# Attention and two mixture-of-experts layers: token rows scattered into one DRAM region per expert, the last rows of an expert in tiles of 64

## The chip, the cores and the metric

The program runs on one core of one Trainium2 chip. A core has TensorE (PE, matrix products, written to the eight banks of PSUM), VectorE (DVE), ScalarE (ACT), GpSimd (POOL) and SyncE (SP), each with its own instruction stream; they meet at semaphores only. All but PE can issue DMAs. The metric is the device time of one execution in microseconds (us), lower is better.

## The reference, cut to what matters

Attention with 4 batches, 8 heads, 768 positions and head size 64, a local window of 96 keys and 8 global keys, gives 3072 token rows of 512. Two layers of experts follow, each with 8 experts of 512 x 1024 and 1024 x 512; every token goes to one expert:

```python
def _moe_ref(x, w_gate, w_output_gate, w1, w2):
    logits = x @ w_gate
    e_idx = np.argmax(logits, axis=1)
    ...
    for e in range(E):
        mask = e_idx == e
        h = np.maximum(x[mask] @ w1[e], 0.0)
        ye = h @ w2[e]
        out[mask] = gate_w[mask, None] * eom[mask, e, None] * ye

def _moe2_ref(x, expert_emb, tau, w1, w2):
    xn = x / (np.linalg.norm(x, axis=-1, keepdims=True) + 1e-06)
    en = expert_emb / (np.linalg.norm(expert_emb, axis=-1, keepdims=True) + 1e-06)
    logits = xn @ en.T / tau
    expert_idx = np.argmax(logits, axis=1)
    ...
        out[mask] = gate_w[mask, None] * (h @ w2[e])
```

`gate_w` is the largest softmax probability of a token, `eom` a sigmoid of a second product. All is float32. With the inputs of this case the experts of the first layer get 455, 416, 361, 397, 367, 410, 395 and 271 tokens, those of the second 445, 228, 374, 430, 340, 278, 299 and 678.

## The kernel before

**Attention.** A batch is six tiles of 128 queries (`j`), a tile two steps (`u`) of four heads. In a step PE makes scores (L1166), DVE adds the bias and takes the maximum (L904), ACT takes the exponent (L709), PE turns the probabilities (L1126), ACT and DVE copy them out of PSUM (L721, L916), and PE multiplies them with the values (L1199). For that last product the two heads of a pair use weights of 64 columns each and write to partitions 0 to 63 and 64 to 127. Two steps later the rows of a tile are turned and normalised into `x_tok` (L876), their 16 gate logits are made (L1141, L883, L887), and ACT's queue writes them to `x_rows` in DRAM (L727). The streams are written out by hand; each engine does the same step `u` in the same order.

**Routing (`route`).** When all 24 tiles are done, DVE finds for all tokens at once the expert, the gate and the rank within the expert, with PE's help (L1217 to L1221), gives each expert whole tiles of 128 slots, and turns the token-to-slot table round with one product per token tile (L1016 to L1023, L1228). In the second layer this waits for all the tiles of the first.

**Experts.** Layer 0 has 29 tiles, layer 1 has 28. A tile on PE is, in this order: `first_product` (L1246, 32 products with 128 moving columns, which the trace lists as 64), `x_tr` of the next tile (L1126, four transposes), `second_product` (L1256, 8 products with 512 moving columns, listed as 16). POOL gathers the 128 rows of a tile by an indirect DMA into `x_g` (L632) as soon as the transposes of the tile before have read it. DVE copies the turned rows (`x_copy`, L1064), scales the result by the gate (`y_scale`, L1075), and in layer 0 makes the eight products of the result with the expert vectors for the next routing (`next_logits`, L1083). ACT applies the ReLU in four pieces (`relu`, L777), and in layer 0 stores the result to `y_rows` (L783) and takes its squares (L785). In layer 1 POOL scatters the result to the output. SP loads the weights of expert e+2 when expert e is through (`load_w`, `load_w2`). Semaphores count tiles; `FIRST` is a credit that they start with.

## Time and profile before

| | |
|---|---|
| three runs, median | 1151.79 us (1151.33 to 1152.15) |
| the profiled execution, its own time | 1149.39 us |
| its span | 1147.0 us |
| PE busy | 1061.3 us, 93% of the span |
| DVE, ACT, POOL busy | 446.4, 262.9, 158.6 us |
| attention, start to its last logits | 0 to 226.0 us |
| first gap, to the first expert product | 226.0 to 264.0 us |
| layer 0, 29 tiles | 264.0 to 684.8 us |
| second gap | 684.8 to 728.4 us |
| layer 1, 28 tiles, and the end | 728.4 to 1147.0 us |

The span is what the engines' records cover; the execution's own time is 2.4 us longer and lies 2.4 us below the median of the runs. A busy share is an average over these stages. PE's matrix products are pipelined, and their recorded ends are modelled, so that the start of the next one says more than the end.

### The profile page before, as it was taken

What the parts mean: (1) busy time and instruction counts of PE and PEld (TensorE: products, weight loads), DVE (VectorE), ACT (ScalarE), POOL (GpSimd) and SP (SyncE); (2) the same over time, 40 slices, a digit from 0 to 9 for tenths busy, and PEclk for the clock granted to TensorE, in tenths of its full rate; (3) what the DMA queues carried; (4) which work ended last, traced back from release to release, by engine and by line L of the source; (5) the groups of instructions that cost most, each with busy time, mean ns of one, the idle gap of its engine ahead of it and who ended that gap; (6) DMA issues with size and microseconds to landing.
All of it is one profiled execution on the core that took longest, in us unless ns stands there. A gap on an engine that the chain in (4) does not pass through costs nothing.

```text
span 1147.0 us, 20797 instructions
## 1 busy us (share of the span) xinstructions
PE 1061.3 (93%) x6936; PEld 806.0 (70%) x6936; DVE 446.4 (39%) x1541; ACT 262.9 (23%) x792; POOL 158.6 (14%) x437
## 2 busy tenths in 40 slices
PE   5999999848999999999999983799999999999995
PEld 4878888646777777777777763577777777777773
DVE  6777777662444444444444449100001111111110
ACT  4677677421111111111111110011111111111110
POOL 2010001001111111111111100122222222222221
PEclk9999999958999999999999995899999999999998
DMA  9865569211151542325151532015523235230110
GB/s 180 183 159 145 132 160 322 99 58 37 37 183 37 183 135 85 131 89 183 37 183 37 183 106 95 28 37 179 181 107 112 98 116 180 90 122 31 37 37 12
DMA packets 119861, 130.30 MB, mean 114 GB/s; under 512 B 80079, under 2 KB 80079, under 8 KB 119696
## 3 DMA queue, kind: packets, MB, share of 16 engines
q1 hardware_dynamic: 103456, 91.24, 26.8%
q0 software_dynamic: 6960, 21.77, 5.8%
q10 hardware_dynamic: 9408, 16.81, 4.0%
q8 instruction: 22, 0.36, 0.1%
q14 instruction: 15, 0.12, 0.0%
HBM read 103.58 MB, written 22.02 MB: 110 GB/s over the span
## 4 chain that ended last, share of the span: by engine, by line
PE 83%; issue 5%; DVE 5%; ACT 4%; DMA 1%; ACTq 1%; POOL 0%; POOLq 0%; DVEq 0%; SPq 0%
PE bank L1246 35%; PE bank L1256 34%; PE bank L1126 6%; PE bank L1199 2%; PE bank L1166 2%; PE bank L1228 2%; PE bank L1141 2%; ACT probs L709 2%; ACT q_t L687 1%; ACT y_two L721 1%; ACTq L727 1%; DVE neg_s L904 0%; DVE nbias L840 0%; DMA n_words<-in_n_local_dram 0%; DMA x_g<-x_rows,gidx 0%
## 5 line engine op out<-in xcount | busy, mean ns | idle before, releaser
L1246 PEld LDWEIGHTS bank<-x_gt,w_sb 128*128 128x128 f32 x3648 | 419.1, 193 | 28.7 <-issue 26.3
L1246 PE MATMUL bank<-x_gt,w_sb 128*128 128x128 f32 x3648 | 419.7, 276 | 1.6 <-DVE x_gt L1064 1.6
L1256 PE MATMUL bank<-w_sb,h_t 128*128 128x512 f32 x912 | 400.8, 592 | 0.0
L1256 PEld LDWEIGHTS bank<-w_sb,h_t 128*128 128x128 f32 x912 | 168.8, 190 | 190.8 <-issue 190.8
L777 ACT ACTIVATE h_t<-bank 128x256 f32<-128x256 f32 x228 | 86.8, 381 | 524.4 <-PE bank L1246 524.4
L1075 DVE TENSOR_SCALAR y_two<-bank,scale_c 128x512 f32<-128x512 f32 x57 | 42.8, 751 | 359.5 <-PE bank L1256 359.5
L586 POOL TENSOR_TENSOR pad_p<-zeros 128x1 f32<-128x1 f32 x196 | 36.9, 188 | 824.8 <-PE bank L1126 470.9
L1064 DVE COPY x_gt<-bank 128x512 f32<-128x512 f32 x59 | 40.8, 691 | 247.2 <-PE bank L1126 247.2
L1083 DVE CUSTOM_DVE_ANT_0 v_win<-y_two,nbias 128x512 f32<-128x512 f32 x174 | 108.8, 687 | 1.2
L785 ACT ACTIVATE y_two<-y_two 128x512 f32<-128x512 f32 x29 | 18.3, 631 | 246.4 <-DVE y_two L1075 246.4
L904 DVE CUSTOM_DVE_ANT_0 neg_s<-bank,nbias 128x256 f32<-128x256 f32 x192 | 70.3, 421 | 7.8 <-issue 6.0
L709 ACT ACTIVATE probs<-neg_s,neg_m 128x256 f32<-128x256 f32 x96 | 47.6, 497 | 51.1 <-DVE neg_m L904 51.1
L1166 PE MATMUL bank<-k_t,q_t 64*128 64x256 f32 x384 | 56.5, 414 | 2.7 <-DVE neg_m L904 1.5
L709 ACT ACTIVATE h_t<-neg_s,neg_m 128x256 f32<-128x256 f32 x96 | 47.7, 498 | 11.4 <-DVE neg_m L904 11.4
L1126 PE MATMUL bank<-ident,x_g 128*128 128x128 f32 x236 | 36.4, 278 | 14.9 <-DMA x_g<-y_rows,gidx 7.5
L1166 PEld LDWEIGHTS bank<-k_t,q_t 64*128 64x128 f32 x384 | 34.3, 192 | 13.7 <-issue 9.9
L1126 PEld LDWEIGHTS bank<-ident,x_g 128*128 128x128 f32 x236 | 28.2, 144 | 15.2 <-issue 15.2
L1083 DVE CUSTOM_DVE_ANT_0 q_in<-y_two,nbias 128x512 f32<-128x512 f32 x58 | 37.7, 687 | 0.0
L632 POOL DMA_INDIRECT x_g<-x_rows,gidx x30 | 31.4, 1045 | 16.0 <-issue 16.0
L632 POOL DMA_INDIRECT x_g<-y_rows,gidx x29 | 30.6, 1055 | 15.7 <-issue 15.7
L1126 PE MATMUL bank<-ident,probs 128*128 128x128 f32 x192 | 27.0, 285 | 5.9 <-ACT y_two L721 5.5
L1126 PEld LDWEIGHTS bank<-ident,probs 128*128 128x128 f32 x192 | 21.3, 144 | 15.6 <-ACT y_two L721 11.7
(176 smaller groups left out, 717.0 us busy)
## 6 DMA issues: line engine op xcount, KB each, us to landing
w_sb<-in_moe_w_dram SPq DMA_DIRECT2D x32, 2048.0 KB, 9.3
y_rows<-y_two ACTq DMA_DIRECT2D x29, 256.0 KB, 2.0
q_in<-in_q_dram SPq DMA_DIRECT2D x24, 256.0 KB, 3.8
k_in<-in_k_dram SPq DMA_DIRECT2D x24, 256.0 KB, 5.0
v_own<-in_v_dram SPq DMA_DIRECT2D x24, 256.0 KB, 3.4
x_rows<-x_tok ACTq DMA_DIRECT2D x24, 256.0 KB, 3.8
v_win<-v_own SPq DMA_DIRECT2D x20, 192.0 KB, 3.4
nbias<-in_moe_expert_emb_dram ACTq DMA_DIRECT2D x1, 2048.0 KB, 7.4
```

The source lines that it names most:

```text
L586: nc.gpsimd.tensor_tensor(pad_p[:, at:at + 1], zeros[:, 0:1], zeros[:, 0:1], ALU.add)
L632: nc.gpsimd.indirect_dma_start(out=x_g[:, :], out_offset=None, in_=src[:, :], in_offset=bass.IndirectOffsetOnAxis(ap=gidx[:, 0:1], axis=0) ...
L709: e_ = nc.scalar.activation(probs_of[u % 2][:, 2 * k + i, :], neg_s[:, k, i, :], ACT.Exp, bias=neg_m[:, i, s % STEPS:s % STEPS + 1], scale ...
L777: nc.scalar.activation(h_t[:, k * FPP:(k + 1) * FPP, :].rearrange("p c t -> p (c t)"), banks[k][:, 0:FPP * P], ACT.Relu).then_inc(L.h, 1)
L904: V.tensor_tensor_reduce(neg_s[:, k, i, :], score_banks[i][:, k * WIN:(k + 1) * WIN], nbias[:, c, 2 * (2 * half + k) + i, :], 1.0, 3e38, A ...
L1064: V.tensor_copy(x_gt[:, :, :].rearrange("p c t -> p (c t)"), banks[5][:, :]).then_inc(L.xt, 1)
L1075: V.tensor_scalar(y_sb, banks[4][:, :], scale_c[:, n, bass.ds(i, 1)], None, ALU.mult).then_inc(L.y, 1)
L1083: t_ = V.tensor_tensor_reduce(dot_out[e], y_sb, emb[:, e * DM:(e + 1) * DM], 1.0, 0.0, ALU.mult, ALU.add, dot[:, e:e + 1])
L1126: t_ = T.transpose(bank[:, c * P:(c + 1) * P], src[:, c * P:(c + 1) * P], ident[:, :])
L1166: m_ = T.matmul(score_banks[i][:, k * WIN:(k + 1) * WIN], q_t[rows, j % 2, 2 * half + k, :], k_t[rows, j % 2, 2 * half + k, :], start=True ...
L1246: m_ = T.matmul(banks[k][:, f * P:(f + 1) * P], w1_sb[:, w1 + c * FF + at:w1 + c * FF + at + P], x_gt[:, c, :], start=(c == 0), stop=(c == ...
L1256: m_ = T.matmul(banks[4][:, :], h_t[:, c, :], w2_sb[:, w2 + c * DM:w2 + (c + 1) * DM], start=(c == 0), stop=(c == FC - 1))
```

## The change

**Where rows go.** `x_rows` and `y_rows` as stores between stages go (`x_rows` stays for general inputs). Each layer has a DRAM region `bins[n]` with N + 128 rows of 532 words per expert: 512 values, then negated scores, and the token's number plus one. During attention, after every third tile, DVE finds the experts of 384 tokens (`group_hot`), PE counts (`group_ranks`), DVE turns that into rows (`group_rows`), and POOL scatters three tiles to `bins[0]` (`scatter_group`). In layer 0 the same is done for each tile of results: scores (`next_scores`), ranks (`rank_rows` on PE), rows (`y_rows`), and a scatter to `bins[1]` (`bin_row`). `route` is replaced by `tables`, 19 small operations on counts.

**Tiles.** An expert has full tiles of 128, and ends in one or two tiles of 64: a remainder of up to 64 tokens is one, more is two. With the counts above layer 0 has 21 full and 11 half tiles, layer 1 has 20 and 11. A half tile makes the first product with the 64 token columns as weights and W1 moving, twice at once in name: the hidden units 0 to 511 to partitions 0 to 63, and 512 to 1023 to partitions 64 to 127. The result has to be turned (`h_turn`), and the second product adds two halves that stand in two halves of the partitions (`high_sums` on ACT, an addition on DVE).

**Gates.** The softmax and the sigmoid of a tile are made in the tile (`gate_exps` on ACT, `gate_weights` on DVE), not ahead. The rows are loaded by SP in two plain DMAs (`load_x`), `x_copy` has moved from DVE to ACT, and so have the weight loads from SP to ACT.

The core of the difference:

```diff
@@ attention, DVE (step) @@
+                t = u - 2 * GROUP - 4
+                if t % (2 * GROUP) == 0 and exists(b, t // (2 * GROUP), 2):
+                    g = t // (2 * GROUP)
+                    dve.wait_ge(lg_copied, since(TPB * b + GROUP * (g + 1)))
+                    group_hot(dve, 2 * b + g, g % 2, TPB * b + GROUP * g)
+                t = t - 1
+                if t % (2 * GROUP) == 0 and exists(b, t // (2 * GROUP), 2):
+                    group_rows(dve, 2 * b + t // (2 * GROUP), t // (2 * GROUP) % 2)
@@ attention, PE (step), ahead of x_transposes @@
+                    pe.wait_ge(lg_copied, since(TPB * b + GROUP * (g + 1)))
+                    group_ranks(pe, 2 * b + g)
@@ group_hot, group_ranks, group_rows, scatter_group @@
+            link(V.tensor_reduce(g_min[:, :], neg, AX.X, ALU.min))
+            link(V.tensor_tensor(g_cmp[:, :, :], neg, wide(g_min[:, :]), ALU.is_equal))
...
+            pe.wait_ge(s_hot, q + 1)
+            pe.wait_ge(s_pos, q + FIRST)
+            T.matmul(banks[5][:, rank_cols], before[:, :], g_hot[:, :, :].rearrange("p t e -> p (t e)"),
+                     start=True, stop=False)
...
+            dve.wait_ge(s_rank, q + 1)
+            V.tensor_tensor(g_cmp[:, :, :], banks[5][:, rank_cols].rearrange("p (t e) -> p t e", e=E),
+                            g_hot[:, :, :], ALU.mult).then_inc(s_route, 1)
...
+                nc.gpsimd.indirect_dma_start(
+                    out=bins[0][:, :], out_offset=bass.IndirectOffsetOnAxis(ap=sc_i[:, j:j + 1], axis=0),
+                    in_=x_tok[:, j, :], in_offset=None,
+                    bounds_check=ZERO - 1, oob_is_err=False).then_inc(x_sc[g], 16)
@@ SP @@
+                def load_x(at, low, high):
+                    sp.wait_ge(L.xt, at + FIRST)
+                    sp.dma_start(x_g[0:UNIT, :], low).then_inc(L.x_ld, 16)
+                    sp.dma_start(x_g[UNIT:P, :], high).then_inc(L.x_ld, 16)
@@ ACT, a full tile: relu_full, gate_exps, x_copy(i + 1), in layer 0 squares @@
+                def x_copy(i):
+                    act.wait_ge(L.x_ld, 32 * i + 32)
+                    act.wait_ge(L.t1, i + 1)
+                    act.wait_ge(L.mm1, MARKS * i + FIRST)
+                    act.wait_ge(L.sc, i + FIRST)
+                    nc.scalar.activation(pay[:, bass.ds(i + 1, 1), :].rearrange("p o c -> p (o c)"), x_g[:, DM:], ACT.Copy)
+                    nc.scalar.activation(x_gt[:, :, :].rearrange("p c t -> p (c t)"), banks[5][:, :],
+                                         ACT.Copy).then_inc(L.xt, 1)
@@ DVE, a tile of layer 0: y_rows, gate_weights, y_full or y_half, next_scores @@
+                def y_rows(i):
+                    dve.wait_ge(L.rank, i + 1)
+                    ids = pay[:, bass.ds(i, 1), 2 * E:2 * E + 1].rearrange("p o c -> p (o c)")
+                    chain(V.tensor_tensor(cmp1[:, :], banks[6][:, 0:E], hot1[:, :], ALU.mult))
+                    chain(V.tensor_reduce(r1[:, 0:1], cmp1[:, :], AX.X, ALU.add))
+                    chain(V.tensor_scalar(r1[:, 1:2], ids, 0.0, OFF, ALU.is_equal, ALU.mult))
+                    V.tensor_tensor(sidx[:, :], r1[:, 0:1], r1[:, 1:2], ALU.add).then_inc(L.pos, 1)
...
+                        dve.wait_ge(L.ex, i + (1 + FIRST))
+                        chain(V.tensor_scalar(g_tmp4[:, 1:2], e_sum[:, :], 1e-9, None, ALU.add))
+                        chain(V.scalar_tensor_tensor(out=g_tmp4[:, 2:3], in0=e_sig[:, :], scalar=1.0,
+                                                     in1=g_tmp4[:, 1:2], op0=ALU.add, op1=ALU.mult))
+                    V.reciprocal(scale[:, :], g_tmp4[:, 2:3]).then_inc(L.sc, 1)
@@ PE @@
-                    with pe.Fori(start, end) as i:
-                        first_product(i, e % 2 * KC * FF)
+                    with pe.Fori(start, mid) as i:
+                        first_full(i, w1)
                         x_tr(i + 1)
-                        second_product(i, e % 2 * FC * DM)
+                        second_full(i, w2)
+                        if n == 0:
+                            rank_rows(i)
+                    with pe.Fori(mid, end) as i:
+                        first_half(i, w1)
+                        x_tr(i + 1)
+                        h_turn(i)
+                        second_half(i, w2)
+                        if n == 0:
+                            rank_rows(i)
...
+                def rank_rows(i):
+                    pe.wait_ge(L.hot, i + FIRST)
+                    pe.wait_ge(L.pos, i + FIRST)
+                    T.matmul(banks[6][:, 0:E], before[:, :], hot1[:, :], start=True, stop=False)
+                    T.matmul(banks[6][:, 0:E], ones[:, :], pre1[:, :], start=False, stop=True).then_inc(L.rank, 1)
...
+                def first_half(i, w1):
+                    pe.wait_ge(L.xt, i + (1 + FIRST))
+                    for k in range(2):
+                        for c in range(KC):
+                            for g in range(2):
+                                at = w1 + c * FF + g * HALF + k * WIN
+                                m_ = T.matmul(banks[k][g * UNIT:(g + 1) * UNIT, 0:WIN], x_gt[:, c, 0:UNIT],
+                                              w1_sb[:, at:at + WIN], start=(c == 0), stop=(c == KC - 1))
+                        m_.then_inc(L.mm1, 1)
...
+                    for c in range(FC // 2):
...
+                        for g in range(2):
+                            at = w2 + (g * FC // 2 + c) * DM
+                            m_ = T.matmul(banks[4][g * UNIT:(g + 1) * UNIT, :], h_t[:, c, g * UNIT:(g + 1) * UNIT],
+                                          w2_sb[:, at:at + DM], start=(c == 0), stop=(c == FC // 2 - 1))
```

The first place is a tile of layer 0 on PE. Before, the end of one full tile and the loop's turn:

```order
L1256 MATMUL bank<-w_sb,h_t 128x512 [waits h_0]
L1256 MATMUL bank<-w_sb,h_t 128x512
L1266 REGISTER_ALU
L1266 COMPARE_AND_BRANCH
```

Now, the same place, where `hot` and `pre` hold which expert the rows of the tile before took and how many rows came before them:

```order
L1423 MATMUL bank<-w_sb,h_t 128x512 [waits h_0]
L1423 MATMUL bank<-w_sb,h_t 128x512
L1398 MATMUL bank<-hot,before 128x8 [waits pos_0,hot_0]
L1399 MATMUL bank<-pre,ones 128x8
L1464 REGISTER_ALU
L1464 COMPARE_AND_BRANCH
```

Two products with 8 moving columns stand behind the second product of every tile of layer 0, and ahead of the next tile's first.

The second place is the same tile on DVE. Before, the loop's top (the copy of the next tile's rows, then the scaling):

```order
L1063 ISA [waits t1_0]
L1064 COPY x_gt<-bank 128x512 [waits mm1_0]
L1068 REGISTER_ALU
L1070 ISA [waits mm2_0]
L1075 ISA [waits sq_0,y_st_0]
L1075 TENSOR_SCALAR y_two<-bank,scale_c 128x512
```

Now, with `rank_0` released by the two products above and `sc_0`, released by the reciprocal, awaited by ACT's copy of the next tile's rows:

```order
L1220 TENSOR_TENSOR cmp<-bank,hot 128x8 [waits rank_0]
...
L1221 TENSOR_REDUCE r<-cmp 128x1 [waits link_0]
...
L1222 ISA [waits link_0]
L1222 TENSOR_SCALAR r<-pay 128x1
...
L1223 TENSOR_TENSOR sidx<-r 128x1 [waits link_0]
...
L1185 TENSOR_SCALAR g_tmp<-e_sum 128x1 [waits ex_0]
...
L1186 SCALAR_TENSOR_TENSOR g_tmp<-e_sig,g_tmp 128x1 [waits link_0]
...
L1188 RECIPROCAL scale<-g_tmp 128x1 [waits link_0]
L1207 TENSOR_SCALAR y_two<-bank,scale 128x512 [waits sq_0,yc_0,mm2_0,sc_0]
```

The copy has gone to ACT, and seven small operations stand ahead of the scaling.

The third place is DVE in the attention's loop, between the end of an even step and the scores of the odd one behind it. Before:

```order
L862 RECIPROCAL inv_sum<-inv_sum 128x8 [waits s_inv]
L902 MEMSET pad_v 128x1 [waits exp_done,qk_done]
```

Now, in the steps in which a group of three tiles is complete:

```order
L1032 RECIPROCAL inv_sum<-inv_sum 128x8 [waits s_inv]
L459 TENSOR_SCALAR x_tok<-iota_f 128x3 [waits lg_copied]
L460 COPY g_pre<-g_pre 128x8 [waits s_route]
L461 TENSOR_REDUCE g_min<-x_tok 128x3 [waits s_route]
L462 TENSOR_TENSOR g_cmp<-x_tok,g_min 128x24 [waits s_route]
L463 TENSOR_TENSOR g_cmp<-g_cmp,iota_f 128x24 [waits s_route]
L465 TENSOR_REDUCE g_min<-g_cmp 128x3 [waits s_route]
L466 TENSOR_TENSOR g_hot<-g_cmp,g_min 128x24 [waits s_route]
L468 TENSOR_TENSOR g_pre<-g_pre,g_hot 128x8 [waits s_route] x3
L1072 MEMSET pad_v 128x1 [waits exp_done,qk_done]
```

Ten operations, each waiting for the one before it, stand ahead of the next step's score operations; three more follow at the end of that step.

## Rows read from the trace of the kernel before

**Rows 1.** The page, part 4: shares of the chain that ended last.
```profile
PE 83%; issue 5%; DVE 5%; ACT 4%; DMA 1%; ACTq 1%; POOL 0%; POOLq 0%; DVEq 0%; SPq 0%
```

**Rows 2.** Chain of waits in order of time (start us, us), two tiles of layer 0.
```profile
612.57 7.14 PE bank L1246 x64
620.15 6.87 PE bank L1256 x16
627.02 7.14 PE bank L1246 x64
```

**Rows 3.** Busy time by stage: attention, the first gap, layer 0.
```profile
core 0: us, PE busy (x) PEld busy (x) DVE busy (x) ACT busy (x) POOL busy (x), PEclk, DMA share, GB/s
...
120.00:180.00 60.00, 58.39 (x588) 48.91 (x584) 44.83 (x196) 41.87 (x140) 6.08 (x21) 1.00 0.61 146
...
226.00:264.00 38.00, 13.49 (x59) 12.84 (x59) 19.41 (x72) 7.86 (x20) 2.09 (x6) 0.50 0.18 70
...
288.00:684.00 396.00, 396.00 (x2283) 289.51 (x2282) 182.27 (x568) 57.85 (x162) 41.58 (x108) 1.00 0.33 115
```

**Rows 4.** Timeline: ACT's copy from PSUM; the first tile's first product.
```profile
119.72 0.57 ACT L687 ACTIVATE q_t<-bank 128x512 f32<-128x512 f32 x1
...
263.97 8.95 PE L1246 MATMUL bank<-x_gt,w_sb 128*128 128x128 f32 x64 [0.78 <-DVE x_gt L1064]
```

**Rows 5.** Timeline: attention's last logits, first gather, and its transposes.
```profile
225.62 0.37 DVE L887 TENSOR_REDUCE logits<-lg_part 128x16 f32<-128x128 f32 x1
...
258.38 1.21 POOL L632 DMA_INDIRECT x_g<-x_rows,gidx  x1 [0.72 <-issue]
...
262.10 1.09 PE L1126 MATMUL bank<-ident,x_g 128*128 128x128 f32 x4 [7.47 <-DMA x_g<-x_rows,gidx]
```

**Rows 6.** Chain and timeline: layer 0's last product, layer 1's first.
```profile
677.95 6.88 PE bank L1256 x16
...
728.36 8.86 PE bank L1246 x64
```

**Rows 7.** Timeline, attention: 64-wide weight loads of sixteen products.
```profile
127.08 0.85 PEld L1199 LDWEIGHTS bank<-probs_t,v_own 128*64 128x64 f32 x16 [0.17 <-issue]
```

**Rows 8.** Timeline: ACT's copy of a quarter of the hidden layer.
```profile
272.95 0.38 ACT L777 ACTIVATE h_t<-bank 128x256 f32<-128x256 f32 x1 [1.40 <-PE bank L1246]
```

**Rows 9.** Timeline (start us, us): a tile's second product ends, the next begins.
```profile
1120.06 7.31 PE L1246 MATMUL bank<-x_gt,w_sb 128*128 128x128 f32 x64
...
1120.47 0.75 DVE L1075 TENSOR_SCALAR y_two<-bank,scale_c 128x512 f32<-128x512 f32 x1 [6.28 <-PE bank L1256]
```

**Rows 10.** Timeline, attention: PE, eight short products and what follows.
```profile
122.19 0.98 PE L1141 MATMUL bank<-gates_h,x_raw 128*128 128x32 f32 x8
...
123.10 0.44 PE L1199 MATMUL bank<-y_two,v_win 128*64 128x128 f32 x4
```

**Rows 11.** Timeline, DVE: small operations that wait for each other, then within a loop.
```profile
123.52 0.28 DVE L883 TENSOR_TENSOR lg_part<-bank,inv_sum 128x128 f32<-128x128 f32 x1
123.95 0.37 DVE L887 TENSOR_REDUCE logits<-lg_part 128x128 f32 x1
...
127.80 0.16 DVE L860 TENSOR_SCALAR inv_sum<-row_sum 128x8 f32<-128x8 f32 x1
127.99 0.20 DVE L862 RECIPROCAL inv_sum<-inv_sum 128x8 f32<-128x8 f32 x1
```

**Rows 12.** The DMA view: issues, KB each, median us from issue to landing.
```profile
y_rows<-y_two ACTq DMA_DIRECT2D x29, 256.0 KB, 2.0
...
x_g<-x_rows,gidx POOLq DMA_INDIRECT x30, 3.6
...
out_dram<-y_two,sidx POOLq DMA_INDIRECT x28, 2.7
```

**Rows 13.** Timeline, attention: DVE's idle ahead of a score step.
```profile
120.89 0.06 DVE L902 MEMSET pad_v<- 128x1 f32 x1 [1.21 <-PE bank L1166]
```

More of the change, by code:

```diff
@@ L558, in _ @@
+                load_x(start, nothing, nothing)
         @block.gpsimd
@@ new lines, in next_scores @@
+                    chain(V.tensor_tensor(pre1[:, :], pre1[:, :], hot1[:, :], ALU.add))
+                    V.tensor_scalar(hot1[:, :], cmp1[:, :], r1[:, 3:4], r1[:, 4:5], ALU.is_equal, ALU.mult)\
+                        .then_inc(L.hot, 1)
+                    dve.wait_ge(L.sq, i + (1 + FIRST))
+                    V.tensor_scalar(y_row[:, DM + E + 1:DM + E + 2], ids, 0.0, None, ALU.add)
+                    V.tensor_copy(y_row[:, DM + E:DM + E + 1], y_norm[:, :]).then_inc(L.row, 1)
+                for e, start, mid, end in expert_spans(dve, n):
+                    for first, last, y_of in ((start, mid, y_full), (mid, end, y_half)):
+                        with dve.Fori(first, last) as i:
+                            here(i)
+                            if n == 0:
+                                y_rows(i)
+                            gate_weights(i, e)
+                            y_of(i)
+                            if n == 0:
+                                next_scores(i)
+                            if no < STEP_LINKS:
+                                dve.sem_inc(L.link, STEP_LINKS - no)
```

828 lines of the change are left out of this document (457 added, 371 removed).

## The prediction

> **What bounds the kernel now.** I read the shares of the chain that ended last first: PE holds 83% of it, DVE and ACT 5% and 4% [rows 1]. The chain in order of time shows how: in both layers it is an unbroken line of first products (7.14 us) and second products (6.87 us), with 0.44 us of transposes between them (612.57 + 7.14 to 620.15), so that a tile takes 14.45 us [rows 2]. The busy times by stage confirm it: in the 396 us of layer 0 shown, PE is busy for all 396, at full clock, while DVE has 182 and ACT 58 [rows 3]. So a microsecond on the other engines costs nothing there unless PE comes to wait for it. In attention PE is busy 58.4 of 60 us, DVE 44.8 [rows 3]. Between the stages lie two gaps. In the first, 38 us from attention's last logits (225.62 + 0.37) to the first product at 263.97 [rows 4, 5], the granted clock is 0.50 of full speed, its lower level of 1.2 GHz [rows 3]; the second runs from 684.83 (677.95 + 6.88) to 728.36, 43.5 us [rows 6].
>
> **Half tiles.** The records of a first product (7.14 us for 64) are 112 ns for 128 columns; of a second product (6.87 for 16) 429 ns for 512 [rows 2]. A half tile has 32 records of 256 columns, then 16 of 512. If both column halves work at once, each pair costs one: 16 x 215 = 3.44 us, and 8 x 429 = 3.43. Attention's value products have just such 64-wide weights: sixteen loads, each with its 128-column product, take 0.85 us, 53 ns each, half of the 112 [rows 7]. So I take the halving. Around it: 0.44 for x's transposes, 0.44 for the turn, and about 1.1 in which PE waits for ACT's two copies of 0.38 [rows 8] with PE's end-to-copy delay of up to 0.41 [rows 9] around the turn. I take 8.4 us; the bounds are 7.75 (nothing waits) and 9.5 (both copies fully exposed, and x late).
>
> The Trainium skill ("TensorEngine Tiling (Array Packing)", Key Properties) says that changing the tiling mode drains the engine. No row shows a price by itself; a half tile changes mode four times, which lies inside my bound of 9.5.
>
> **The new wait of layer 0.** This is the largest term. `rank_rows(i)` stands behind the second product of tile i on PE. `y_rows(i)` on DVE waits for it; `gate_weights(i)` stands behind `y_rows(i)` on DVE, although its exponents are long there, and releases `sc`; ACT's `x_copy(i + 1)` waits for `sc`; and PE's next first product waits for that copy. It is a ring without slack, once per tile. Step by step, from the end of the second product:
> - the two rank products, four records: eight short ones take 0.91 us (122.19 to 123.10), so 0.46 [rows 10];
> - PE's end to DVE's start: 0.41 for a long product [rows 9]; I take 0.35;
> - seven small DVE operations. Start to start such pairs take 0.19 us, and 0.43 where an address is computed in between and the first lasts 0.28, hence 0.15 of pause [rows 11]. I take 0.25 each, 1.75;
> - ACT: 0.10 to wake, 0.19 for the small copy ahead, 0.57 for the 128x512 copy from PSUM [rows 4]: 0.86;
> - ACT's end to PE's start 0.06 (0.78 of wait less DVE's copy, which lasts 0.69, rounded) [rows 4].
> Sum 3.5 us. Bounds: 2.8 (0.28 of delay, 0.19 for each operation, 0.75 on ACT) and 4.2 (0.41, 0.30, 1.1). Over 32 tiles 112 us (90 to 134). The eight products with the expert vectors, POOL's scatter and the squares follow in the shadow of the next tile: they take some 10.7 us of a turn of at least 11.9.
>
> **Layer 0** before: 29 x 14.45 = 419.1. After: 21 full x 14.45 = 303.5, 11 half x 8.4 = 92.4, and 112: 507.9. **+88.8.**
>
> **Layer 1.** Here no rank products exist, and DVE's `gate_weights(i)` (some 17 small operations, about 4 us) starts when x is copied and ends within the tile; in a half tile it leaves under 1 us of slack, and a loss of up to 1 us for each of 11 is in the range. 20 x 14.45 + 92.4 = 381.4 against 28 x 14.45 = 404.6: **-23.2.**
>
> **Loading x.** SP issues the two plain loads only when the copy before has read `x_g`; they are wanted 7.14 us later, or 3.44 in a half tile. A plain 256 KB transfer lands in 2.0 us, an indirect gather in 3.6 [rows 12]. Two issues and 2.0 just fit 3.44. While weights stream (two transfers back to back behind an expert's end) a load is later, once per expert. I take +2 (0 to +20).
>
> **Attention.** Eight groups put ten chained operations (10 x 0.22 = 2.2 us) at the end of an even step and three (0.9 us) at the end of the odd one. DVE's idle ahead of the score operation there is 1.21 us [rows 13], so about 1.0 us is passed on at once, and again some of the three; PE has 0.5 us more products and waits for `hot`. I take 2.0 for each of the seven groups that lie inside attention: **+14** (0, if all is absorbed, to +25, if nothing is). The eighth lies in the gap. ACT's stores to `x_rows` go; they were off the path. POOL's three indirect DMAs per group (about 1.2 us each [rows 5]) lie between the key copies of tiles that are needed two steps later, and cost nothing; if that cover were gone, POOL would hold back PE by up to 4 us per group.
>
> **First gap.** From the last logits: last group 2.3 on DVE, 1.3 for PE at half clock, 1.1 for the rows (230.7), counts 2 to 3 us later with a jump to new code, `tables` 19 x 0.2 = 3.9 (237.5), SP's four fills and table loads 3, x 2.5, transposes 1.09 [rows 5], the two copies 0.9: 20 us for 38. The last scatter runs beside it. **-18** (-12 to -22).
>
> **Second gap.** From the last second product: 3.5 of ring are counted above; scaling and addition of a half tile to 5.2, eight expert products 5, eight small operations 2, two pairs of products 1.3, `tables` 3.9, fills and loads 5.5, transposes and copies 2, one jump 2: 27. Less 3.5 and against 43.5: **-19.5** (-13 to -24).
>
> **The end.** The last tile is a half one, with ACT's copy and DVE's addition ahead of the scaling: **+2.** Moving weight loads to ACT, and the table load in its first loop, lie under a second product, 6.87 us in which ACT has nothing due.
>
> **Sum**, against the profiled execution: 88.8 - 23.2 + 2 + 14 - 18 - 19.5 + 2 = +46. Span 1147.0 + 46 = 1193; its own time 2.4 more, 1195.5. That execution lies 2.4 us below the median of the runs, so I predict 1197 us.
>
> **Rivals.**
> *The ring is short enough (faster).* Without the ring the sum is 1197 - 112 = 1085, so the change wins if a turn of the ring costs less than (1151.8 - 1085) / 32 = 2.1 us. The point that decides is whether DVE's seven operations take 0.19 us or less and PE's end is seen at once: 0.4 of products, 0.2, 7 x 0.1, 0.7 on ACT make 2.0. For it: recorded ends overlap the next start. Against: starts of waiting pairs are never nearer than 0.19 [rows 11], so 2.8 stands as the bound. With 2.0 and an absorbed attention: 1197 - 48 - 14 = 1135 us.
> *The clock falls in each turn (slower still).* PE idles about 3 us in each turn. After 0.78 us of direct waiting at the end of the first gap, with little work before it, the first tile's 64 records took 8.95 us for 7.14, and the granted clock was at its lower level [rows 2, 3, 4]. If each turn did that, 32 x 1.8 = 58 us more: 1255. Against it: attention has waits too and keeps 1.00 [rows 3], and a tile of layer 0 is over four fifths dense products.
> The Trainium skill ("TensorE: Matmul & The Clock Gate", HAM oscillation) describes kernels in which a wait for data before each group of products starts each group at half clock; by that rule the price would be these 58 us. No row shows an idle time of 3 us amid dense work.
> *The column halves don't work side by side.* Then a half tile costs 6.9 us more, 22 of them 151: 1348, and the change doesn't do what it says. [Rows 7] speak against it.
>
> **Numbers.** The forecast 0.74 (its own range 1165 to 1225: ring +-22, attention +-12, gaps +-10, x up to +18, not all at once), the falling clock 0.13, the fast ring 0.08, no concurrency 0.02, others on either side 0.03. The range to 8 in 10: 1158 to 1255. Slower by more than 0.2% (what a measurement of this kernel can tell from no change) 0.90, within 0.02, faster 0.08.
>
> **What would show it.** In the profile after: PE idle before L1413 and L1434 put down to ACT's `x_gt`, some 3 us x 32, in layer 0 alone, and DVE's wait for the bank of L1399; chain shares of DVE and ACT well above 5% and 4%; first products of half tiles (L1434) spanning 3.4 us; granted clock 1.00 within layer 0 (the clock rival: below 0.95); DVE's last logits at about 240 us, first products of the layers about 20 and 27 us after what came before; a full tile of layer 1 still 14.45 us. It is wrong if layer 0's full tiles come at 16 us or less, or if x's loads end the waits.

## The result: 5.7% slower, and the profile after

The changed kernel takes **1216.7 us** (median of 4 runs, 1215.6 to 1220.4) against 1152.0 (4 runs, 1151.3 to 1152.7): a ratio of 1.057, interval 1.054 to 1.059. The forecast was 1197 with a range of 1158 to 1255, and slower with 0.90. So direction and range held, and the time came 20 us above the forecast. The profiled execution has a span of 1213.7 us.

First the page of the changed kernel: busy time of the engines, TensorE's busy tenths and its granted clock in 40 slices, and the shares of the chain that ended last (the row that answers to [rows 1]).

```profile
PE 1039.7 (86%) x6870; PEld 746.8 (62%) x6870; DVE 607.0 (50%) x2639; ACT 352.1 (29%) x1130; POOL 182.3 (15%) x377
...
PE   5999999738889888888888988639999999999995
...
PEclk9999999859999999999899899959999999999998
...
PE 42%; issue 33%; DMA 9%; DVE 5%; POOL 4%; ACT 4%; SPq 1%; POOLq 1%; ACTq 0%; another core or an unknown queue 0%; DVEq 0%
```

PE's row reads mostly 8 where layer 0 runs (slices 10 to 25), and 9 all through layer 1. In [rows 1] PE held 83% of the chain. Now it holds 42%, but this is not the ring's mark. Through most of layer 0 the chain now runs along POOL: its scatters (`bins<-q_in`), and between them idle time that the profile calls "issue". The first experiment's kernel, in which the ring is gone, has much the same shares:

```profile
PE 45%; issue 28%; DMA 10%; DVE 5%; POOL 5%; ACT 4%; SPq 1%; POOLq 1%; ACTq 0%; DVEq 0%
```

So one of the forecast's signs did not come (shares of DVE and ACT "well above 5% and 4%": they are 5% and 4%), and the chain decides nothing here. What decides is the idle time of PE itself. The costliest groups say what PE waits for (busy, mean ns, idle before, releaser).

```profile
L1413 PE MATMUL bank<-x_gt,w_sb 128*128 128x128 f32 x2624 | 323.2, 287 | 49.3 <-ACT x_gt L892 49.3
...
L1220 DVE TENSOR_TENSOR cmp<-bank,hot 128x8 f32<-128x8 f32 x33 | 5.5, 167 | 219.3 <-PE bank L1399 219.3
...
L1434 PE MATMUL bank<-w_sb,x_gt 128*64 128x256 f32 x704 | 87.4, 405 | 26.1 <-ACT x_gt L892 26.1
...
L891 ACT ACTIVATE pay<-x_g 128x20 f32 (+1 forms) x65 | 14.2, 219 | 296.2 <-DVE scale L1188 252.8
```

PE waits 75 us for ScalarE's `x_gt`, ScalarE for VectorE's `scale`, and VectorE for PE's rank product: the ring that the prediction named. One turn of it, in the timeline (start, duration, and in brackets the idle time ahead of the instruction):

```profile
376.18 0.28 PE L1398 MATMUL bank<-hot,before 128*128 128x8 f32 x2
376.32 0.37 PE L1399 MATMUL bank<-pre,ones 128*128 128x8 f32 x2
376.73 0.17 DVE L1220 TENSOR_TENSOR cmp<-bank,hot 128x8 f32<-128x8 f32 x1 [8.01 <-PE bank L1399]
...
377.43 0.16 DVE L1223 TENSOR_TENSOR sidx<-r 128x1 int32<-128x1 f32 x1
...
377.91 0.16 DVE L1188 RECIPROCAL scale<-g_tmp 128x1 f32<-128x1 f32 x1
...
378.26 0.22 ACT L891 ACTIVATE pay<-x_g 128x20 f32 x1 [8.43 <-DVE scale L1188]
378.39 0.58 ACT L892 ACTIVATE x_gt<-bank 128x512 f32<-128x512 f32 x1
...
379.02 1.16 PE L1413 MATMUL bank<-x_gt,w_sb 128*128 128x128 f32 x8 [2.33 <-ACT x_gt L892]
```

From 376.18 (second product over) to 379.02 it takes 2.84 us. VectorE's seven operations begin at 376.73 and the last ends at 378.07: 1.34 us or 0.19 each, where 0.25 each was forecast.

The stages of the changed kernel, as busy times by window (PE, PEld, DVE, ACT, POOL, then the granted clock, DMA share and GB/s), answer to [rows 3]:

```profile
262.00:780.00 518.00, 439.41 (x2508) 306.55 (x2508) 271.19 (x1064) 112.57 (x362) 81.32 (x122) 0.95 0.26 86
780.00:812.00 32.00, 3.16 (x14) 2.60 (x13) 12.96 (x58) 2.13 (x5) 3.63 (x6) 0.55 0.58 183
813.00:1200.00 387.00, 383.33 (x2296) 259.54 (x2296) 132.76 (x659) 80.41 (x258) 45.53 (x120) 0.99 0.31 104
```

In layer 0 PE is now busy 439 of 518 us (before: all of it), at a clock of 0.95 and not 1.00. (The forecast would have taken a clock below 0.95 as the mark of its rival; this lies on the border.) In layer 1 nothing is lost. Its timeline shows a full tile, a half tile, and the next full one:

```profile
844.10 7.31 PE L1413 MATMUL bank<-x_gt,w_sb 128*128 128x128 f32 x64
...
851.68 7.03 PE L1423 MATMUL bank<-w_sb,h_t 128*128 128x512 f32 x16
858.64 3.67 PE L1434 MATMUL bank<-w_sb,x_gt 128*64 128x256 f32 x32
...
863.68 3.65 PE L1455 MATMUL bank<-w_sb,h_t 128*64 128x512 f32 x16 [0.33 <-ACT h_t L913]
867.26 7.41 PE L1413 MATMUL bank<-x_gt,w_sb 128*128 128x128 f32 x64
```

32 records of 256 columns take 3.6 us, where one after the other they would take 6.9 (32 x 215 ns, an estimate from [rows 2]). So the two column halves work at once, and the half tile takes 8.62 us from start to start (8.4 was forecast).

The six stretches of the two profiled executions, from starts and ends in the timelines:

| stretch | before | after | change | forecast |
|---|---|---|---|---|
| start to last logits | 226.0 | 236.4 | +10.4 | +14 |
| first gap | 38.0 | 26.0 | -12.0 | -18 |
| layer 0, first product to end of last second product | 420.9 | 517.3 | +96.4 | +87.3 |
| second gap | 43.5 | 33.3 | -10.2 | -16 |
| layer 1 | 406.3 | 387.1 | -19.2 | -23.2 |
| end | 12.4 | 13.6 | +1.2 | +2 |
| span | 1147.0 | 1213.7 | +66.6 | +46 |

(The stages are rounded one by one. The forecast counted the last turn of the ring, 3.5 us, with layer 0. The table has it in the second gap.)

Layer 0 needs a closer look, since two errors cancel in it. Where the clock stays up, a full tile takes 17.40 us from start to start and a half one at least 11.56 (up to 12.3). That is 2.95 above the 14.45 and 3.0 above the 8.56 of layer 1, where 3.5 was forecast. But besides the first tile, which takes 20.06 us right behind the gap, nine of the 21 full tiles take 18.8 to 20.4 us, typically 19.03, and four of the eleven half ones some 13.3 us. The windows around one such start (342.60, after 2.42 us of waiting for `x_gt`):

```profile
340.00:342.60 2.60, 0.18 (x3) 0.09 (x2) 1.06 (x7) 0.73 (x3) 0.91 (x2) 1.00 0.00 0
342.60:345.00 2.40, 2.40 (x13) 2.40 (x14) 1.57 (x4) 0.98 (x2) 0.30 (x1) 0.59 0.49 128
345.00:348.00 3.00, 3.00 (x22) 3.00 (x22) 3.00 (x9) 0.69 (x3) 1.30 (x2) 0.76 0.80 201
```

The granted clock drops from full speed to its lower level of 1.2 GHz right behind the wait and is 1.00 again in the window from 350 to 361. So the forecast's rival, the clock that falls in each turn, came true in 13 of the 31 turns.

The first gap in the timeline: the last group's hot chain begins, the tables are ready, SyncE's fills, the first x load, its transposes, the first product.

```profile
236.43 0.17 DVE L459 TENSOR_SCALAR x_tok<-iota_f 128x3 f32<-128x3 f32 x1
...
246.86 0.19 DVE L1131 CAST tab<-tab_f 128x56 int32<-128x56 f32 x1
...
248.21 4.99 SPq L609 DMA_DIRECT2D bins<-none  x4
256.82 0.55 SPq L672 DMA_DIRECT2D x_g<-bins  x1
...
260.45 1.08 PE L1288 MATMUL bank<-ident,x_g 128*128 128x128 f32 x4 [19.50 <-DMA x_g<-bins]
...
262.38 1.01 PE L1413 MATMUL bank<-x_gt,w_sb 128*128 128x128 f32 x3 [0.84 <-ACT x_gt L892]
```

The gather that took the end of this gap before [rows 5] is gone. In its place SyncE stands from 247.05 to 256.82 in four fills and nine loads of table entries: 9.8 us, of which the forecast had 3.

### The profile page after: what moved, and what is told of

Its sections match the earlier page's. It is cut to its first block, busy times and chain, and to the rows that moved or that the text cites. A ratio compares the mean times of both kernels' runs of the same rounds, so it can differ in the third digit from the quotient of the medians.

```text
span 1213.7 us, 24789 instructions
## 1 busy us (share of the span) xinstructions
PE 1039.7 (86%) x6870; PEld 746.8 (62%) x6870; DVE 607.0 (50%) x2639; ACT 352.1 (29%) x1130; POOL 182.3 (15%) x377
## 4 chain that ended last, share of the span: by engine, by line
PE 42%; issue 33%; DMA 9%; DVE 5%; POOL 4%; ACT 4%; SPq 1%; POOLq 1%; ACTq 0%; another core or an unknown queue 0%; DVEq 0%
PE bank L1413 13%; PE bank L1423 12%; DMA bins<-q_in,sidx 8%; PE bank L1288 5%; PE bank L1455 3%; PE bank L1434 3%; POOL q_in L774 3%; PE bank L1330 2%; PE bank L1368 2%; POOL pad_p L724 2%; PE bank L1304 1%; ACT probs L837 1%; DVE neg_s L1074 1%; ACT y_two L849 1%; ACT q_t L815 1%
## 5 line engine op out<-in xcount | busy, mean ns | idle before, releaser
L1413 PE MATMUL bank<-x_gt,w_sb 128*128 128x128 f32 x2624 | 323.2, 287 | 49.3 <-ACT x_gt L892 49.3
L1413 PEld LDWEIGHTS bank<-x_gt,w_sb 128*128 128x128 f32 x2624 | 317.6, 203 | 63.3 <-ACT x_gt L892 51.9
L1423 PE MATMUL bank<-w_sb,h_t 128*128 128x512 f32 x656 | 288.3, 592 | 0.0
L1423 PEld LDWEIGHTS bank<-w_sb,h_t 128*128 128x128 f32 x656 | 121.4, 190 | 137.3 <-issue 137.3
L900 ACT ACTIVATE h_t<-bank 128x256 f32<-128x256 f32 x164 | 62.7, 384 | 298.3 <-PE bank L1413 290.5
L1434 PE MATMUL bank<-w_sb,x_gt 128*64 128x256 f32 x704 | 87.4, 405 | 26.1 <-ACT x_gt L892 26.1
L1434 PEld LDWEIGHTS bank<-w_sb,x_gt 128*64 128x64 f32 x704 | 52.0, 145 | 60.7 <-ACT x_gt L892 27.1
L1455 PE MATMUL bank<-w_sb,h_t 128*64 128x512 f32 x352 | 80.4, 598 | 7.3 <-ACT h_t L913 7.3
L1288 PE MATMUL bank<-ident,x_g 128*128 128x128 f32 x260 | 41.2, 282 | 37.6 <-DMA x_g<-bins 20.4
L1455 PEld LDWEIGHTS bank<-w_sb,h_t 128*64 128x64 f32 x352 | 23.3, 136 | 50.3 <-issue 37.7
L1230 DVE CUSTOM_DVE_ANT_0 k_in<-y_two,nbias 128x512 f32<-128x512 f32 x64 | 48.4, 791 | 0.0
```

What stands on the lines that cost most here:

```text
L900: nc.scalar.activation(h_t[:, k * FPP:(k + 1) * FPP, :].rearrange("p c t -> p (c t)"), banks[k][:, 0:FPP * P], ACT.Relu).then_inc(L.h, 1)
L1230: t_ = V.tensor_tensor_reduce(dot_out[e], y_sb, emb[:, e * DM:(e + 1) * DM], 1.0, 0.0, ALU.mult, ALU.add, dot[:, e:e + 1])
L1288: t_ = T.transpose(bank[:, c * P:(c + 1) * P], src[:, c * P:(c + 1) * P], ident[:, :])
L1413: m_ = T.matmul(banks[k][:, f * P:(f + 1) * P], w1_sb[:, w1 + c * FF + at:w1 + c * FF + at + P], x_gt[:, c, :], start=(c == 0), stop=(c == ...
L1423: m_ = T.matmul(banks[4][:, :], h_t[:, c, :], w2_sb[:, w2 + c * DM:w2 + (c + 1) * DM], start=(c == 0), stop=(c == FC - 1))
L1434: m_ = T.matmul(banks[k][g * UNIT:(g + 1) * UNIT, 0:WIN], x_gt[:, c, 0:UNIT], w1_sb[:, at:at + WIN], start=(c == 0), stop=(c == KC - 1))
```

## The experiments

Eight kernels, in two sets. Each shared its chip with runs of the kernel before (1151.3 us in the first set, 1150.7 in the second).

### The scale ahead of the rank step

```diff
 with dve.Fori(first, last) as i:
     here(i)
+    gate_weights(i, e)
     if n == 0:
         y_rows(i)
-    gate_weights(i, e)
```

> VectorE computes a tile's scale (L1185 to L1188) ahead of the rank step y_rows instead of behind it, so that ScalarE may copy the next tile's x_gt while the second product runs. Nothing is left out. Theory (the ring rank, y_rows, scale, pay, x_gt is what holds TensorE 2.84 us ahead of each first product of layer 0, and its idle time is what lets the clock fall in some turns): full tiles of layer 0 go from 17.4 or 19.0 us to about 14.6, the granted clock of layer 0 from 0.94 to over 0.98, and 21 x 2.84 = 60 us and some 9 x 1.63 = 15 us go, so about 1142 us, 75 below the changed kernel. The half tiles stay near 11.5 us, since from rank to rank VectorE needs 0.5 + 1.2 (y_rows) + 1.2 (y) + 6.4 (dots) + 1.7 (hot) = 11 us for each. Rival (x_gt was only the last of several waits that come at about the same time, hot or the landing of the x rows next): full tiles stay above 16.5 us and the time above 1185. Other rival: the half tiles fall to 8.6 us too, which gives 1110.

Measured: **1131.2 us** (1129.2 to 1133.9), 0.983 of the kernel before (0.982 to 0.985): 85.5 us below the changed kernel, from one call put elsewhere. The timeline of a full tile's second half and the next start:

```profile
285.31 0.16 DVE L1188 RECIPROCAL scale<-g_tmp 128x1 f32<-128x1 f32 x1
...
285.78 0.58 ACT L892 ACTIVATE x_gt<-bank 128x512 f32<-128x512 f32 x1
...
290.42 0.37 PE L1399 MATMUL bank<-pre,ones 128*128 128x8 f32 x2
...
290.65 1.58 PE L1413 MATMUL bank<-x_gt,w_sb 128*128 128x128 f32 x12
...
290.83 0.17 DVE L1220 TENSOR_TENSOR cmp<-bank,hot 128x8 f32<-128x8 f32 x1 [5.36 <-PE bank L1399]
```

The copy of `x_gt` starts 4.9 us before PE wants it, and the product at 290.65 follows the rank products with no wait. Full tiles take 14.90 to 14.97 us (14.45 and the rank products), apart from the first (16.26) and two behind half tiles (16.54), and PE's waits for `x_gt` fall from 75.4 to 12.6 us in the whole kernel. The ring and what hung on it were the loss. It is 11 us more than expected: the half tiles, for which the expectation had no gain, take 10.6 to 11.3 us where they took 11.6 to 13.3, and attention ended 2.9 us earlier in this execution (see the scatters below). The half tiles don't come down to layer 1's 8.6, as expected: VectorE's own turn of rank step, scaling, eight dots and hot chain is as long. There the clock still falls, three times in layer 0. The start of one half tile, and the window that begins just ahead of it (granted clock third from the end):

```profile
314.61 0.39 PE L1398 MATMUL bank<-hot,before 128*128 128x8 f32 x2 [0.31 <-DVE hot L1243]
...
316.57 5.36 PE L1434 MATMUL bank<-w_sb,x_gt 128*64 128x256 f32 x32 [1.34 <-ACT x_gt L892]
```

```profile
316.00:320.00 4.00, 3.43 (x18) 2.04 (x20) 2.93 (x10) 1.88 (x6) 1.21 (x2) 0.62 0.42 135
```

The lower clock came after a wait of 1.3 us here: the same 32 products took 5.36 us for 3.6. It does not come each time. A full tile at 543.67, behind a wait of 1.36 us, took 14.91.

### The ranks ahead of the second product

```diff
 first_full(i, w1)
 x_tr(i + 1)
+if n == 0:
+    rank_rows(i)
 second_full(i, w2)
-if n == 0:
-    rank_rows(i)
```

(and likewise in the half tile's program, ahead of `second_half`.)

> TensorE computes the ranks of a tile between its first and its second product instead of behind the second; VectorE's order stays as in the changed kernel. Nothing is left out. The ranks need hot, which came 9.8 us behind the second product's end and would come about 8.5 us behind it without the rank step ahead of y. Theory (ring as in the other run, hot as the next wait): x_gt no longer waits, TensorE waits for hot instead, about 1 us per full tile (8.5 less 7.1 and 0.4) and about 3.4 us per half tile (8.5 less 5.1): full tiles 15.5 us, half tiles 12 us, time about 1216.7 - 21 x 1.9 - 15 = 1162 us. Rival (hot is not near): 14.6 and 8.6 us, time about 1110. Rival (the wait of a few us per turn is put elsewhere and stays as long): full tiles 17.4 us, no change within 10 us.

Measured: 1196.6 us (1196.3 to 1196.9), 20 less than the changed kernel and 35 more than the theory gave. Most full tiles came as expected, 15.6 to 15.7 us. The half tiles did not: 15.1 to 15.5 us (one 13.9), where 12 was expected. In eight of the eleven the wait for `hot` is the 3.4 us of the expectation, but it stands in the middle of a half tile; in the second of two half tiles it is 4.7 us. Timeline of one of each, and the granted clock of the window behind the first wait:

```profile
316.39 0.60 PE L1398 MATMUL bank<-hot,before 128*128 128x8 f32 x2 [3.39 <-DVE hot L1243]
...
317.34 6.53 PE L1455 MATMUL bank<-w_sb,h_t 128*64 128x512 f32 x16
...
333.08 0.39 PE L1398 MATMUL bank<-hot,before 128*128 128x8 f32 x2 [4.73 <-DVE hot L1243]
```

```profile
316.40:320.00 3.60, 3.60 (x12) 1.73 (x14) 1.11 (x8) 0.67 (x2) 1.07 (x2) 0.50 0.01 2
```

The whole second product ran at 1.2 GHz, 6.53 us for 3.65. In the second of two half tiles it took about 5.1. So a wait that is moved and not removed was paid twice, once as idle time and once in clock. Over the eleven half tiles the second products took 26 us more than at full clock. The longer waits of three of them, and the seven full tiles behind half tiles, which waited 1.43 us for `hot` in place of 0.45 and took 16.70, account for about 11 more. Together that is the 35 us that the theory had missed, and a little over.

### The wait filled with products

```diff
+def busy():
+    for m in range(4):
+        T.matmul(banks[7][:, 0:WIN], ident[:, :], iota_f[:, 0:WIN], start=True, stop=True)
...
     rank_rows(i)
+    busy()
```

> The changed kernel with four added products of the identity by 256 columns into a bank that layer 0 doesn't use, behind each tile's ranks in layer 0 (about 4 x 0.43 = 1.7 us, inside the 2.84 us in which TensorE waits); their results are used by nothing. Theory (the tiles of 19.0 us are tiles after whose wait the granted clock had fallen, because TensorE was idle 2.3 us per turn): the clock of layer 0 goes from 0.94 to over 0.98, every full tile takes 17.4 us, and the time falls by 9 x 1.63 for full tiles and some 5 for the half tiles, 20 us in all, to 1197. Rival (those tiles are long because of a transfer, x rows or weights, and the lower clock is a sign of it and not the cause): nothing changes within 3 us. Second rival (the added products delay the ranks' readers): each turn gets longer, time above 1220.

Measured: **1191.3 us** (1190.2 to 1192.0), 25 us less than the changed kernel, from work that nothing uses. The timeline of one turn, then layer 0's window to 747 us of this kernel and of the changed one:

```profile
353.15 1.97 PE L1403 MATMUL bank<-iota_f,ident 128*128 128x256 f32 x8
355.63 2.61 PE L1417 MATMUL bank<-x_gt,w_sb 128*128 128x128 f32 x21 [0.51 <-ACT x_gt L892]
```

```profile
262.00:747.00 485.00, 462.44 (x2688) 322.65 (x2687) 264.75 (x1038) 109.27 (x352) 78.30 (x120) 1.00 0.27 91
```

```profile
262.00:747.00 485.00, 411.42 (x2348) 288.93 (x2349) 253.91 (x996) 106.14 (x340) 75.79 (x114) 0.94 0.27 88
```

PE's idle time per turn falls to 0.5 us, the clock stays at 1.00, and the full tiles take 17.4 to 17.7 us, the first one apart. Layer 0 lasts 496.2 us for 517.3. The falling clock had cost 21 us. The rest of the 25 is attention's end, which came 2.6 us earlier in this execution (below). Both rivals fall: the long tiles were no sign of a transfer.

### The scatters spread

```diff
 window(b, 0)
-scatter_group(pool, hold_pool, 2 * b - 2, 0)
-for j in range(1, 4):
-    window(b, j)
+scatter_begin(pool, hold_pool, 2 * b - 2)
+scatter_tile(0, 0)
+window(b, 1)
+scatter_tile(0, 1)
+window(b, 2)
+scatter_tile(0, 2)
+window(b, 3)
 landed(pool, 0, b)
...
```

> In the attention's loop POOL issues its three row scatters of a group one at a time between the window copies instead of three back to back (the last batch's groups stay as they are). Nothing is left out. Theory (the attention lasts 10.4 us longer partly because POOL is held about 3 us by three scatters of 1 us each and the window copies behind them come late, as the VectorE waits of 2.2 to 2.9 us ahead of some score steps, 1.2 before, suggest): last logits 3 to 6 us earlier, time 1211 to 1214. Rival (the attention is longer by the 2 us that VectorE spends on each group's hot chain and rows, 7 groups of them on the path, and POOL is not on it): no change within 1.5 us. Second rival: slower by 1 to 3 us, since each group's landing is waited for later.

Measured: 1215.1 us (1212.6 to 1220.0) against 1216.7 (1215.6 to 1220.4): no difference that these runs can tell. The trace is clearer than the times. The rows of `x_tok` written per query tile come in the same rhythm (8.18, 8.82, 9.54 us and so on) in this kernel and in the ones with the scale moved and with the waits filled, whose attention is that of the changed kernel. The last group's hot chain starts at 233.4 to 233.8 us in all three. The changed kernel's own profiled execution is the odd one, 236.43, although its attention code is the same as in two of them. My theory, which read a cause out of that one trace, falls. Spreading POOL's scatters gains nothing against the kernels that leave them together.

### The hot chain twice

```diff
-link(V.tensor_reduce(g_min[:, :], neg, AX.X, ALU.min))
...
-link(V.tensor_tensor(g_hot[:, :, :], g_cmp[:, :, :], wide(g_min[:, :]), ALU.is_equal))
+for _ in range(2):
+    link(V.tensor_reduce(g_min[:, :], neg, AX.X, ALU.min))
...
+    link(V.tensor_tensor(g_hot[:, :, :], g_cmp[:, :, :], wide(g_min[:, :]), ALU.is_equal))
```

> The kernel with the scale ahead of the rank step, in which VectorE computes each attention group's hot rows twice: five more small operations of 0.20 us, 1.0 us for each of the 8 groups, with the same values. Nothing is left out. Theory (a group's chain of small operations stands on the path of the attention, and the prediction's 2.0 us per group was too much only because some of it is taken up by waits): attention longer by 0.8 to 1.0 us per group, 6 to 8 us, time 1138. Rival (what makes the attention's group of three query tiles 26.6 us instead of 26.0 is not that chain but the late start of something behind it): less than 0.3 us per group, time within 2.5 us of 1131.2.

Measured: 1141.6 us (2 runs, 1141.5 and 1141.6), 10.4 above the kernel with the scale moved. The timeline shows two query tiles' rows with the group's chain between them:

```profile
165.73 0.68 DVE L1047 TENSOR_TENSOR x_tok<-bank,inv_sum 128x512 f32<-128x512 f32 x1
176.45 0.68 DVE L1047 TENSOR_TENSOR x_tok<-bank,inv_sum 128x512 f32<-128x512 f32 x1
```

That is 10.72 us; with the single chain the same two stand at 162.29 and 171.94, 9.65 apart. So the added 1.0 us is passed on whole (1.2 per group on the mean of six), and the last group, among attention's thinner last steps, cost 3.7 (20.1 for 16.4 us to the last row); hence 10.4 and not the 6 to 8 expected. Yet the chain that the change brought, 2.2 us and 0.9 us for the rows, costs much less than itself. Over the 18 query tiles in the middle of attention it costs 4.2 us (160.3 for 156.1), 0.7 per group; in the changed kernel's own trace 5.4, 0.9 per group. So the first two microseconds fit into waits that VectorE had anyway, and what was added beyond them was paid in full.

### The half tiles in the full program

```diff
 with pe.Fori(mid, end) as i:
-    first_half(i, w1)
+    first_full(i, w1)
     x_tr(i + 1)
-    h_turn(i)
-    second_half(i, w2)
+    second_full(i, w2)
```

(and the full tile's program on ScalarE and VectorE; the scale is ahead of the rank step.)

> The kernel with the scale ahead of the rank step, in which half tiles run through the full tile's program (64 of the 128 columns of x are of the zero rows). Nothing is left out. It prices the part of the change that the column halves are. Theory (a half tile costs 10.9 us in layer 0 and 8.56 in layer 1, a full one 14.93 and 14.5): 11 x 4.0 + 11 x 5.9 = 109 us more than 1131.2, so about 1240 us. Rival (the pace of some half tiles is set by loads of weights and of x rows, which stay): 10 to 30 us less than that.

Measured: 1247.1 us (2 runs, 1245.3 and 1248.8), 116 above 1131.2, where 109 was expected. The timeline of two half tiles in this form:

```profile
306.74 7.39 PE L1413 MATMUL bank<-x_gt,w_sb 128*128 128x128 f32 x64
...
321.64 7.39 PE L1413 MATMUL bank<-x_gt,w_sb 128*128 128x128 f32 x64
```

14.90 us for 10.9, and in layer 1 14.45 for 8.56, which gives 44 and 65; the other 7 us are a colder first tile (17.8), some single longer ones (15.4 to 16.8) and a second gap longer by about 3. The layers now have 32 and 31 tiles, where there were 29 and 28: six more tiles cost 6 x 14.45 = 87 us, and the column halves give back 109 to 116. Nearly all of that surplus is layer 1's (65 for 43 us); in layer 0 the halves only pay for their three tiles (44 for 43), since VectorE holds them at 10.9 us.

### The fills off SyncE's path

```diff
-for e in range(0, E, 2):
-    fill_bin(sp, n, e)
+fill_bin(sp, n, 0)
...
 fulls = entry(sp, n, FULLS, e, 1, NT)
-halves = entry(sp, n, HALVES, e, 1, 2)
 high_row = entry(sp, n, HIGH_ROW, e, UNIT, ZERO)
-half_row = entry(sp, n, HALF_ROW, e, P, ZERO)
-mid = entry(sp, n, MID, e, 2 * e + 1, TILES)
...
     with sp.Fori(0, fulls) as k:
...
+halves = entry(sp, n, HALVES, e, 1, 2)
+half_row = entry(sp, n, HALF_ROW, e, P, ZERO)
+mid = entry(sp, n, MID, e, 2 * e + 1, TILES)
...
+for e in range(2, E, 2):
+    fill_bin(pool, n, e, L.fillp)
```

The last two lines stand on POOL, ahead of its loop over the tiles.

> The kernel with the scale ahead of the rank step (1131.2 us), and besides: SyncE issues only expert 0's fill ahead of the first x load, POOL issues those of experts 2, 4 and 6, and SyncE loads the three table entries that only the half tiles need behind the loop of the full tiles. Nothing is left out. Theory (in each of the two gaps the first x load is late because SyncE stands in fills and table loads from 245.3 to 254.0 us): three fills of 1.2 us and three table loads of 0.7 us leave the path, 5.8 us, of which some may be given back to the landing of expert 0's fill (about 2 us behind its issue): 4 to 5.8 us per gap, 8 to 11.5 us in all, time 1120 to 1123. Rival (the first product waits for something else that comes at about the same time, the scattered rows' landing or ScalarE's own fills): less than 2 us per gap, time above 1127.

Measured: **1121.6 us** (5 runs, 1120.6 to 1123.9), 9.6 less than with the scale moved alone. First gap, timeline:

```profile
244.60 4.52 ACTq L610 DMA_DIRECT2D bins<-none  x4
245.01 0.58 SPq L610 DMA_DIRECT2D bins<-none  x1
248.07 0.56 SPq L672 DMA_DIRECT2D x_g<-bins  x1
...
254.37 7.82 PE L1419 MATMUL bank<-x_gt,w_sb 128*128 128x128 f32 x44 [0.84 <-ACT x_gt L898]
```

The load issues at 248.07, not 254.03, and the first product follows 5.1 us earlier (254.37 for 259.49). In the second gap the load issues 4.3 us behind the start of the last table operation, where it was 9.6, and the gap is 4.4 us shorter. The two gaps give 9.6 us together. The profiled executions themselves differ by 5.9 us only, since in this one layer 0 is 2.7 us longer (first tile 17.56 us for 16.26, and three full tiles of 16.54 for two); that the medians differ by just what the gaps give is in part chance.

### The half tiles fed

The kernel above, with three of the added products behind the ranks of each half tile of layer 0.

> As the kernel with the fills moved, and three products of the identity by 256 columns (1.3 us, results not used) behind the ranks of each half tile of layer 0. Theory (a half tile of layer 0 has 32 first products in 5.36 us at a granted clock of 0.62, against 3.45 us at full clock, since TensorE waits 1.3 us for x_gt and before it for hot): the first products come back to about 3.5 us where the wait was, up to 1.9 us for each of the 11 half tiles, but VectorE's own turn of about 10 us is a floor, so some 5 to 10 us in all. Rival (VectorE sets the half tiles' pace anyway): no change within 2 us. Second rival (the added products push the ranks' successors): up to 11 x 1.3 us = 14 us slower.

Measured: **1119.8 us** (5 runs, 1117.8 to 1119.9), 1.8 less than without them, a small step whose runs lie just clear of the other's. The products did come back to full clock:

```profile
313.43 3.67 PE L1444 MATMUL bank<-w_sb,x_gt 128*64 128x256 f32 x32
```

But the half tiles still take 10.8 to 11.0 us: VectorE sets their pace, as the rival said. What went are the full tiles of 16.5 us behind some of them (three between 379 and 613 us before, none now). This is the fastest version, 0.973 of the kernel before (0.971 to 0.974).

## Why the forecast was 20 us low

**The ring** was found where it was and by the right steps, and was given 3.5 us a turn; it takes 2.95 (17.40 less 14.45). By the turn at 376.18, most of the over-estimate is VectorE's seven operations (1.34 us for 1.75), and the rest is the rank products with PE's end to VectorE's start (0.55 for 0.81). That is 32 x 0.55 = 18 us too much. Moving one call took the ring out and 85 us with it, so this term is shown, not argued.

**The clock** is the step that failed. The forecast put its cost at nothing: it had layer 0 at a granted clock of 1.00 and gave the falling clock 0.13, although no row of before had 3 us of waiting amid dense work to judge by. The trace after has 31 waits of 2.3 to 2.7 us inside layer 0, and behind 13 of them the tile took 1.4 us or more too long. The price is 21 us of layer 0 (517.3 to 496.2 us when the waits were filled), neither nothing nor the rival's 58. The Trainium skill ("TensorE: Matmul & The Clock Gate", HAM oscillation) describes a kernel in which the wait for data ahead of each group of products lets the clock fall every time; its waits are about 3 to 5 us, longer than these. The trace agrees that waits make the clock fall, here 2.3 us already, and not that it happens every time. With the wait in the middle of a half tile (3.4 or 4.7 us, the ranks ahead of the second product) the clock did fall each time, and the second product took 5.1 to 6.5 us for 3.65.

**The two gaps** were each 6 us longer than forecast (26.0 and 33.3 for 20 and 27). The term too small was SyncE's: "fills and table loads 3" and 5.5 in the second gap, where 9.8 and 9.5 us passed between the tables and the first x load. Moving part of it gave back 9.6 us in the two gaps together. The x load was too small as well: 3.6 and 3.7 us from its issue to the transposes, where the first gap had 2.5 and the second had no such term. The forecast's jumps to new code had no row to show them. In the first gap 2.0 us do pass between PE's counts (at 240.97) and the first table operation, within the "2 to 3" of that term; in the second the tables follow VectorE's last rank operation at once, and no jump of 2 us shows. (The first gap's terms add up to 19 us, not 20, and the second's to a change of -20, not -19.5.)

**Attention** was forecast at +14 and measured at +10.4 in this execution, and at +7.3 to +8.1 in six others with the same attention code. 2.0 us per group was too much: 0.7 to 0.9. The chain's cost is not proportional; the forecast took about 1.0 us as hidden, and it was about 2. About 1.9 of the +7.5 us have nothing to do with it: the first query tile's rows are that much later (38.1 us for 36.2), ahead of any group.

**Half tiles** were right: 8.4 forecast, 8.51 to 8.62 measured in layer 1, both halves at once. Layer 1 gained 4.0 us less than forecast. It lasted 5.7 us more than the forecast's 381.4: 2.3 of a cold first tile (16.71), 11 x 0.18 of half tiles, and 0.1 for each side on which a full tile has a half one for a neighbour (14.55, and 14.65 between two). The same stage of the kernel before lasted 1.7 us more than its 404.6, mostly by its own cold first tile (16.01), which the forecast left out too. The Trainium skill ("TensorEngine Tiling (Array Packing)", Key Properties) says that changing the mode drains the engine; between a full tile and a half one the price in this trace is at most about 0.1 us per change.

**Loading x** (+2) cost less than 1 us of direct waiting. **The end** (+2) was +1.2.

In sum, against the forecast: layer 0 +9.1 (ring -17, fallen clock and cold first tile +26, half tiles +2, x -2), gaps +12, layer 1 +4.0, attention -3.6, end -0.8; together 20.7, which is 1213.7 less 1193. That the total came this near is in part luck: the 17 us too much for the ring covered two thirds of the 26 too little for the clock and the cold first tile. The "faster" rival had its point of decision at 2.1 us per turn, and the measured 2.95 lies on the slower side. That point was itself too high: with the kernel without the ring at 1131 us, only (1151 - 1131) / 32 = 0.6 us more per turn would have eaten the gain. The forecast's own time without any ring was 1085; the kernel without it takes 1131. Of the 46 us between them, the rank products of the full tiles, which the 3.5 us had included, are 21 x 0.45 = 9, the half tiles of layer 0, at 10.9 us (rank products and VectorE's pace) and not 8.4, are 27, the gaps are 12, layer 1 is 4, and attention gives back 6, which closes it to within a few microseconds.

## What to carry to other kernels

When a change adds a step between two engines, follow the wait in program order through every engine before coding it: here `y_rows` stood ahead of a computation that didn't need it, and turned a gain of 1.7% into a loss of 5.7%. A wait that PE meets once per turn cost its length and, in some turns, 1.4 to 2.9 us more in clock; until it was removed, filling it with useless products was cheaper than leaving it. And a chain of small operations was free up to the engine's own waits and cost its full length beyond, so price the next microsecond, not the average one. Last, check that the chain of waits passes through the place you explain: here its shares looked like the ring and stayed when the ring was gone.

## What the hardware showed that I had not expected

- The granted clock fell after a wait of 2.3 to 2.4 us amid dense work in some turns and not in others of the same length (2.33 us ahead of the tile at 734.48, which lost 1.6 us, and 2.33 ahead of the one at 379.02, which lost nothing), and in the kernel with the scale moved after 1.34 us in one place and not after 1.36 in another. What decides it, the runs don't show.
- The same attention code ran in two rhythms: per three query tiles 26.5 to 27.1 us, as 8.2, 8.8, 9.6 (six traces) or as 9.7, 9.4, 7.6 (the changed kernel's), with attention's end 3 us apart. With one trace of each kernel it is open whether this changes from execution to execution or goes with the rest of the program. A difference of 3 us in one stage of one trace is no finding.
- On SyncE, the load of a table entry from memory into a register took 0.5 to 0.8 us from start to start, and a fill with its table load about 1.5 (fills at 249.80, 251.26 and 252.72): nine such loads and four fills were 9.8 us on the path, on an engine for which the page shows no busy time.
